# Keys of two head pairs with exchanged halves, and short score products, in a fused attention and feed-forward kernel

## The reference

```python
for t in range(S):                       # S = 768, state (B, H, 48, 48)
    cur = einsum('bhd,bhe->bhde', u * kt, vt)
    y[:, :, t] = einsum('bhd,bhde->bhe', rt, state + cur)
    state = wt[..., None] * state + einsum('bhd,bhe->bhde', kt, vt)
x = y as (1536, 384)
x = elu(x @ w_in) @ w_out                # 384 -> 2048 -> 384
out = sum over 4 experts e of p[:, e] * (relu(x @ w1[e]) @ w2[e])
```

## Time and profile before

| what | before |
|---|---|
| median of 3 runs | 646.91 us (646.85 to 646.93) |
| the profiled execution | 646.69 us, its span 644.9 us |
| granted TensorE clock | 1.000 of 2.4 GHz over the span |
| PE busy | 638.4 us (99%) x5046 |
| DVE busy | 418.6 us (65%) x786 |
| ACT busy | 237.1 us (37%) |
| POOL busy | 296.0 us (46%) |
| scores, L1199 | 320 matmuls, 11.0 us busy, 275 ns each in the record |

### The profile page before, as it was taken

One profiled execution on the slowest core, in us unless ns is written; L12 is line 12 of the kernel. 1 busy time (PEld: TensorE's weight loads), 2 busy tenths in 40 slices (PEclk: granted clock), 3 DMA queues, 4 the chain that ended last, 5 costly groups with the idle time before them and its releaser, 6 DMA issues.

```text
span 644.9 us, 13796 instructions
## 1 busy us (share of the span) xinstructions
PE 638.4 (99%) x5046; PEld 591.5 (92%) x5046; DVE 418.6 (65%) x786; ACT 237.1 (37%) x557; POOL 296.0 (46%) x370
## 2 busy tenths in 40 slices
PE   8999999999999999999999999999999999999998
PEld 5998999877788888999999999999999999999997
DVE  7889999865357666565655555565656565656564
ACT  4785555655455554222222222222222222222221
POOL 5897424420499999996029900029900018000000
PEclk9999999999999999999999999999999999999999
DMA  8954454300000233000012100013100011001011
GB/s 322 403 193 137 138 183 164 124 11 1 1 2 1 73 98 99 27 1 1 1 50 99 50 1 0 1 49 99 50 1 0 0 50 50 0 1 49 0 50 50
DMA packets 19043, 42.34 MB, mean 66 GB/s; under 512 B 2608, under 2 KB 8752, under 8 KB 18992
## 3 DMA queue, kind: packets, MB, share of 16 engines
q1 hardware_dynamic: 18704, 41.23, 18.6%
q10 hardware_dynamic: 288, 0.39, 0.2%
HBM read 37.16 MB, written 4.46 MB: 65 GB/s over the span
## 4 chain that ended last, share of the span: by engine, by line
PE 90%; DVE 4%; POOL 3%; issue 1%; DMA 0%; ACT 0%; DVEq 0%; POOLq 0%
PE bank L1365 29%; PE bank L1366 29%; PE bank L1367 29%; POOL w_lo L546 3%; PE bank L1199 1%; PE bank L1278 1%; DVE fr L863 1%; PE bank L1290 1%; DVE fr L882 1%; DVE att L921 0%; DMA rkw<-rkw_dram 0%; DVE w_lo L966 0%; DVE bank L996 0%; PE bank L1232 0%; PE bank L1298 0%
## 5 line engine op out<-in xcount | busy, mean ns | idle before, releaser
L1365 PE MATMUL bank<-x_lo,w_hi 128*128 128x256 f32 (+2 forms) x416 | 138.1, 332 | 0.5 <-POOL w_lo L546 0.3
L1366 PE MATMUL bank<-x_hi,w_lo 128*128 128x256 f32 (+2 forms) x416 | 135.2, 325 | 0.0
L1367 PE MATMUL bank<-x_hi,w_hi 128*128 128x256 f32 (+2 forms) x416 | 135.2, 325 | 0.0
L1366 PE MATMUL bank<-w_hi,g_lo 128*128 128x384 f32 x384 | 129.6, 338 | 0.0
L1367 PE MATMUL bank<-w_hi,g_hi 128*128 128x384 f32 x384 | 129.3, 337 | 0.0
L1365 PE MATMUL bank<-w_lo,g_hi 128*128 128x384 f32 x384 | 129.0, 336 | 0.0
L826 ACT ACTIVATE g_hi<-bank 128x512 fp32r<-128x512 f32 x96 | 57.5, 598 | 144.3 <-DVE bank L1052 122.4
L1365 PEld LDWEIGHTS bank<-x_lo,w_hi 128*128 128x128 f32 x416 | 78.2, 188 | 10.4 <-issue 2.5
L1367 PEld LDWEIGHTS bank<-x_hi,w_hi 128*128 128x128 f32 x416 | 78.3, 188 | 7.4
L1366 PEld LDWEIGHTS bank<-x_hi,w_lo 128*128 128x128 f32 x416 | 78.3, 188 | 7.1
L1045 DVE TENSOR_TENSOR u_sum<-p_copy,bank 128x256 f32<-128x256 f32 x56 | 23.6, 421 | 92.1 <-ACT p_copy L750 91.3
(11 more groups left out here) (134 smaller groups left out, 1258.8 us busy)
## 6 DMA issues: line engine op xcount, KB each, us to landing
raw<-w_dram SPq DMA_DIRECT2D x48, 384.0 KB, 3.7
rkw<-rkw_dram SPq DMA_DIRECT2D x10, 772.5 KB, 4.5
tok<-tok_dram SPq DMA_DIRECT2D x10, 576.0 KB, 5.9
k_blocks_dram<-k_blocks SPq DMA_DIRECT2D x8, 256.0 KB, 4.1
kt_sb<-k_blocks_dram SPq DMA_DIRECT2D x32, 64.0 KB, 2.0
out_dram<-acc SPq DMA_DIRECT2D x10, 192.0 KB, 1.9
rkw<-rkw_dram SPq DMA_DIRECT2D x2, 512.0 KB, 4.4
rkw<-rkw_dram SPq DMA_DIRECT2D x2, 260.5 KB, 3.3
```

The lines of the kernel that those rows point to most:

```text
L1365: pe.matmul(out, wh, ml, start=start, stop=False, skip_group_check=shared)
L1366: pe.matmul(out, wl, mh, start=False, stop=False, skip_group_check=shared)
L1367: return pe.matmul(out, wh, mh, start=False, stop=stop, skip_group_check=shared)
```

## The change

The tokens of a chunk are not in plain order for all heads any more. For chunks 2 to 11 the key and value rows (and the r rows of the bonus) of pairs 0 and 1 have their two halves of 64 exchanged on the partitions: `load_tok` does it while loading, with three DMAs in place of one, in pieces of 192 elements (768 bytes). `turn_blocks` does it for the turned keys, with three transposes in place of one: 128, 128 and 256 elements per partition. The bonus diagonal takes three selects (256, 256 and 512 elements) in place of two of 512, and both masked copies wait for all three. The places of pairs in `att` become 0, 2, 1, 3, and the mask becomes two masks side by side, one with exchanged rows, loaded by two DMAs more.

The scores of a chunk are now made of 8 long products (the earlier 64 keys, all 128 queries) and 8 short ones (the later 64 keys, the later 64 queries only). For pairs 0 and 1 the earlier keys go to the upper column half of the array, for pairs 2 and 3 to the lower one. The order is: pair 0 long (both heads), pair 0 short, pair 2 long, pair 2 short, pair 1 long, pair 1 short, pair 3 long, pair 3 short; so on each column half long and short products are in turn.

```diff
-        const = sb("const", [P, NCONST])
+        const = sb("const", [P, 3 * P])
...
+        def exchanged(p):
+            return p < PAIRS // 2
+        def place(c, p):
+            return p if c < FIRST else p % 2 * 2 + p // 2
...
-            return 2 * (c + 1 - FIRST)
+            return 3 * (c + 1 - FIRST)
...
-                sp.dma_start(tok[c % DEEP][:, :], tok_d[c]).then_inc(s_tok[c % DEEP], 16)
+                def columns(t, first):
+                    return t.rearrange("p (s n) -> p s n", s=3)[:, :, first:first + DM // 2]
+                here, there = tok[c % DEEP], tok_d[c]
+                sp.dma_start(columns(here[0:HALF, :], 0), columns(there[HALF:CH, :], 0)).then_inc(s_tok[c % DEEP], 16)
+                sp.dma_start(columns(here[HALF:CH, :], 0), columns(there[0:HALF, :], 0)).then_inc(s_tok[c % DEEP], 16)
+                sp.dma_start(columns(here[:, :], DM // 2), columns(there, DM // 2)).then_inc(s_tok[c % DEEP], 16)
...
-            sp.dma_start(const[:, :], const_d).then_inc(s_const, 16)
+            sp.dma_start(const[:, P:3 * P], const_d[:, C_MASK:C_MASK + 2 * P]).then_inc(s_const, 16)
...
             load_tok(3)
+            for rows, others in ((slice(0, HALF), slice(HALF, CH)), (slice(HALF, CH), slice(0, HALF))):
+                sp.dma_start(const[rows, 0:P], const_d[others, C_MASK:C_MASK + P]).then_inc(s_exchanged, 16)
...
-                for o in range(2):
-                    pool.affine_select(att[:, o, :, :], heads[:, o, :].unsqueeze(2).broadcast_to([P, PAIRS, CH]),
...
+                diagonal(0, 0, HALF, HALF)
+                diagonal(0, HALF, HALF, 0)
+                diagonal(1, 0, CH, 0)
...
-                dve.transpose(k_blocks[:, :, :].rearrange("q t (a j) -> q t a j", a=PAIRS),
-                              raw_k(c).rearrange("q (a t i) -> q t a i", a=PAIRS, i=STRIP)).then_inc(s_kb, 1)
+                strips = raw_k(c).rearrange("q (a t i) -> q t a i", a=PAIRS, i=STRIP)
+                turned = k_blocks[:, :, :].rearrange("q t (a j) -> q t a j", a=PAIRS)
+                dve.transpose(turned[:, 0:2, 0:2, :], strips[:, 2:4, 0:2, :]).then_inc(s_kb, 1)
+                dve.transpose(turned[:, 2:4, 0:2, :], strips[:, 0:2, 0:2, :]).then_inc(s_kb, 1)
+                dve.transpose(turned[:, :, 2:4, :], strips[:, :, 2:4, :]).then_inc(s_kb, 1)
...
-                    dve.wait_ge(s_diag, diagonal_done(c) - 1 + o)
-                    dve.copy_predicated(att[:, o, :, :], masks.bitcast(I32), found).then_inc(s_att, 1)
+                    dve.wait_ge(s_diag, diagonal_done(c))
+                    found = banks["x"][o][:, :].rearrange("p (a t) -> p a t", a=PAIRS // 2)
+                    dve.copy_predicated(att[:, o, :, :].rearrange("p (a b) t -> p a (b t)", b=2),
+                                        both_masks.unsqueeze(1).broadcast_to([P, PAIRS // 2, 2 * CH]).bitcast(I32),
+                                        found).then_inc(s_att, 1)
...
+                def block(p, o, later, first, count):
+                    rows, at = slice(64 * o, 64 * o + D), HALF * (later != exchanged(p))
+                    out = place(c, p) * CH + first
+                    return pe.matmul(banks["x"][o][at:at + HALF, out:out + count],
+                                     k[rows, p * CH + HALF * later:p * CH + HALF * later + HALF],
+                                     q[rows, p * CH + first:p * CH + first + count], start=True, stop=True)
+                for p in range(PAIRS // 2):
+                    for one in (p, p + PAIRS // 2):
+                        for o in range(2):
+                            block(one, o, 0, 0, CH)
+                        for o in range(2):
+                            ins = block(one, o, 1, HALF, HALF)
```

More of the change, by code:

```diff
@@ L518, in bonus_terms @@
             def bonus_terms(c):
-                landed(pool, s_tok, c)
+                tok_landed(pool, c)
                 t = tok[c % DEEP]
@@ L699, in copy_odd @@
             def copy_odd(c):
-                landed(act, s_tok, c)
+                tok_landed(act, c)
                 need(act, s_py, c - 1)
@@ L941, in bonus_v @@
                 dve.wait_ge(s_pb, c + 1)
-                landed(dve, s_tok, c)
+                tok_landed(dve, c)
                 sums = banks["bonus"][:, 0:H].unsqueeze(2).broadcast_to([P, H, D])
@@ L1189, in scores @@
                 q, k = q_of(c), k_of(c)
[L1190 to L1194, removed]
-                            ins = pe.matmul(banks["x"][o][:, cols], k[rows, cols], q[rows, cols], start=True, stop=True)
[L1196 to L1200, removed]
+                if c < FIRST:
+                    for p in range(PAIRS):
+                        cols = slice(p * CH, (p + 1) * CH)
+                        for o in range(2):
+                            rows = slice(64 * o, 64 * o + D)
+                            ins = pe.matmul(banks["x"][o][:, cols], k[rows, cols], q[rows, cols], start=True, stop=True)
+                    ins.then_inc(s_px, 1)
+                    return
+                def block(p, o, later, first, count):
[8 more added lines that the diff above has]
+                            block(one, o, 0, 0, CH)
+                        for o in range(2):
+                            ins = block(one, o, 1, HALF, HALF)
                 ins.then_inc(s_px, 1)
@@ L1217, in update @@
                 pe.wait_ge(s_att, c * 2 + 2)
-                landed(pe, s_tok, c)
+                tok_landed(pe, c)
                 v = v_of(c)
@@ L1289, in values_even @@
                     columns = STRIP // 2 if b % 3 == 1 else STRIP
-                    pe.matmul(strip_of(yt, b)[0:columns], v[:, first:first + columns], att[:, 0, p, :],
+                    pe.matmul(strip_of(yt, b)[0:columns], v[:, first:first + columns], att[:, 0, place(c, p), :],
                               start=False, stop=True, skip_group_check=True)
             def odd_strip(c, yt, b):
-                return pe.matmul(strip_of(yt, b), v_of(c)[:, b * STRIP:(b + 1) * STRIP], att[:, 1, b // 3, :],
+                return pe.matmul(strip_of(yt, b), v_of(c)[:, b * STRIP:(b + 1) * STRIP], att[:, 1, place(c, b // 3), :],
                                  start=False, stop=True, skip_group_check=True)
             def odd_end(c, yt, b):
-                return pe.matmul(strip_of(yt, b), v_odd[:, c % 2, b // 3, :], att[:, 1, b // 3, :],
+                return pe.matmul(strip_of(yt, b), v_odd[:, c % 2, b // 3, :], att[:, 1, place(c, b // 3), :],
                                  start=False, stop=True, skip_group_check=True)
```

33 lines of the change are left out of this document (22 added, 11 removed).

## The result

| | before | after |
|---|---|---|
| median | 646.92 us (646.85 to 646.99, 6 runs) | **649.98 us** (649.08 to 650.31, 6 runs) |
| ratio | | 1.0045, 95% interval 1.0034 to 1.0055 |
| the profiled execution | 646.69 us, span 644.9 | 649.08 us, span 647.4 |

The changed kernel is 3.1 us slower, where 0.7 us less was forecast. The profiled executions differ by 2.4 us, their spans by 2.5.

A forecast was written before the change was run, and what follows sets the result against it. The prediction took POOL, then DVE, as bounds, PE from 68.78 us; DVE's lead was thin until chunk 8. PE 0.11 us late after chunk 7, less 0.84 for chunks 8 to 11, gave -0.73: 646.2 us, range 645.3 to 647.5.

The forecast's parts named there:

- The loads ... Taken at nothing: Split token loads: added issues and 0.3 us more engine time per load are covered by slack, so cost nothing.
- The place: Checked chunk 9's load and the updates of chunks 6 and 7 (0.4 and 0.5 us in hand); at the start only bytes count.
- The price of a packet: Token loads on the 16 DMA engines: 25 ns per 512 bytes, 111 ns per 2.74 KB; 0.3 us more per load.
- The issues: SP queue: 0.47 us per issue, 0.94 more per token load, covered at chunk 9; six start weight slices delayed up to 1.9.
- Rival C: Keys' road through DRAM becomes the bound at updates of chunks 6 and 7: PE 0.74 late, about 646.9 to 647; chance 0.06.
- The short products: Scores on PE: four long and four short passes per array part save 0.21 us a chunk; ends 0.24 and nothing.
- rival A: DVE's addition is covered after all; seven scores on PE gain 0.21 each, 1.47 us, giving 645.4; chance 0.18.
- B: Scores on PE: a short product frees its array part only after the earlier long one; no saving, 647.2; chance 0.18.
- D: Scores on PE: column halves of unequal lengths do not run side by side; +3.8 us, 650.7; chance 0.07.
- DVE's transposes: Turned keys on DVE, chunks 2 to 9: three transposes for one add 0.15 us a chunk; ends 0.05 and 0.38.
- DVE's other addition: Masked copies and bonus sum cost DVE nothing; the third select costs POOL about 0.1 us, covered by 1.8 in hand.
- The range: Whole kernel: 645.3 to 647.5 us, leaving out the slowest rival and the dearest case of the no-saving one.

The follow-up runs named there:

- small_rows: The kernel before with each token load from chunk 2 on still one DMA, but in 768-byte rows, no further loads; 647.18 us, ratio 1.0006.
- by_tensor: The kernel before with each token load in three DMAs (r, k, v) over all 128 partitions, 1536-byte rows, plus two mask-row loads; 647.05 us, ratio 1.0000.
- rows_split: The kernel before with each token load in three DMAs of whole 4608-byte rows over 64, 32, 32 partitions, plus two mask-row loads; 653.55 us, ratio 1.0112.
- three_loads: The kernel before with each token load in three DMAs of 768-byte pieces, not exchanged, plus two mask-row loads; 650.57 us, ratio 1.0059.
- early_split: The kernel before with three-DMA token loads for chunks 2 and 3 alone, plus the two mask-row loads; 649.08 us, ratio 1.0038.
- late_split: The kernel before with three-DMA token loads in 768-byte rows for chunks 4 to 11 alone; 647.56 us, ratio 1.0008.
- host_laid: The changed kernel with tokens and mask laid out exchanged in DRAM by the host, each token load one DMA again; 646.91 us, ratio 1.0000.

## Why the prediction was wrong

**The step that failed is "The loads ... Taken at nothing".** It cost 3.64 us alone. It failed in two of its terms, and a third was mis-sized:

- *The place.* It looked for the cost at chunks 6 to 9 and dismissed the start, "their queue is then ten us deep, so only bytes count". The start carries 2.25 of it. The queue was deep, but PE was not far behind it: before, too, the chain ran through low parts of weights up to 37 us. Of the two further places, PE waited at the update of chunk 2, which the forecast did not look at, and at that of chunk 5.
- *The price of a packet.* "By the first rate a `tok` load takes 1.8 us of the 16 engines, by the second 1.5": the second rate came from DMAs over all partitions. The first came from the narrow reads of `kt_sb`, which are not slow, so it gave no warning either. For 768 packets on 16 engines 1.8 and 1.5 us mean 38 and 31 ns. The first is what a full DMA takes (40 in small_rows); those of a split load took 53, or 2.5 us of the 16 engines for a load.
- *The issues.* 0.47 us was the price of whole loads. The split ones take 0.55 to 0.61 each and the two of the mask 2.57 together, so that the six slices began 4.3 us later and not "up to 1.9" (its own six issues at 0.47 us make 2.8). The number of issues is not what costs: by_tensor has as many, its slices begin at 19.77, 2.3 us later than before, and it loses 0.06 us. There the forecast's argument, that only the queue's content counts, holds.

**Rival C** had the right mechanism, the keys' road as the bound, with a chance of 0.06; its place (the updates of chunks 6 and 7) and its price (0.74) were wrong, and its time of 646.9 to 647 with them. It was not the slower-side rival it should have been.

**The short products: right.** 0.21 us for a chunk was forecast, and a stretch of 0.87 to 0.92 with its tail; 1.10 - 0.90 = 0.20 was measured in the stretch. Their whole gain by themselves is 1.16 us: 0.19 to 0.21 at six of the seven chunks and nothing at chunk 8, from a start 0.29 us late; rival A's 1.47 was on the high side. Rivals B (a stretch of 1.10) and D (a longer one) are refuted by the same rows, and so is, for this case, the rule of the Trainium skill (TensorE: Matmul & The Clock Gate, what overlaps and what doesn't) that matmuls end strictly in program order, as far as B drew from it: short products on one part of the array do not wait for long ones on another. As ends of matmuls are modelled in these records, this rests on the starts: the next product starts 0.83 us after the scores do (88.46 to 89.29), for 1.03 before (85.21 to 86.24).

**DVE's transposes: right.** 0.15 forecast, 0.13 measured (0.75 or 0.76 for 0.63), +0.18 us for the kernel. The 0.31 that the prediction worked out from the Trainium skill (VectorE: DVE Perf Modes, the section on the TRN2 errata) is not seen.

**DVE's other addition: missed.** "The masked copies and the bonus sum keep their element counts: nothing" held, but the third select was priced at 0.1 us on GpSimd with 1.8 us of cover. It takes 0.15 there, and DVE pays it: the scan beside GpSimd's next product grows from 1.53 to 1.68. A chunk therefore cost DVE 0.28 and not 0.15. Hence the entry for chunks 5 to 7 was later, and chunk 8, taken as free, met the low part at 118 us, where 0.2 us were in hand and not the 1.4 of the queries. Forecast for everything but the loads -0.73, measured -0.02.

**The range** ended at 647.5 since the loads had no upper end beyond C. No large DMA over a part of the partitions in a full queue stood in the trace of before, and the bounds for it were taken from loads of another kind. That an operation has no near row was said for the short products, and not for this.

## What to carry to other kernels

A large DMA over one half of the partitions is not half a DMA: its packets were 1.5 times as long as those over all of them (308 ns for 205), at the start 1.9 times (341 for 180), and in a stretch where the queue is full this delays everything queued behind, whoever needs it. With the long wait that it caused in rows_split TensorE's clock fell too. An exchange of partition halves is better laid in DRAM, or made where queue and consumers have slack. And an operation added on GpSimd can be paid by DVE: look at what runs beside it, not only at its own slack.

## What the runs showed of the hardware

- Where a DMA's partitions lie decides the time of its packets: 205 ns for 4608 bytes over all 128, 308 with cuts at 64 and 96, 245 with cuts at 32 and 96 (means from 60 to 107 us). Reads of 512 bytes over 32 partitions, with the engines mostly idle, stay at 27 to 29 ns.
- Row size matters less: six times the packets of 768 instead of 4608 bytes in one full DMA cost 0.35 us in all, within the interval of nothing.
- A scan of 520 elements on DVE takes 1.53 or 1.68 us depending on whether GpSimd's product starts 0.17 us ahead of it or with it, and 1.24 with no product beside it; why the order matters was not tried.
- TensorE's granted clock fell from 2.4 to 1.2 GHz near the end of a wait of 2.92 us in rows_split, and at 47.17 us in the changed kernel, behind a wait of 1.67 and shorter ones; products of 256 columns then start 0.21 us apart for 0.12. In the profile of three_loads, with waits of 1.07 and 1.92 us, it stayed at 2.4 there.
- What remains open: early_split and late_split sum to 2.98 of 3.64 us, and the parts three_loads and host_laid to 3.62 where the change cost 3.06. Each wait takes over slack that another leaves, and lower clocks stand in some runs and not in others; these differences were not followed further.
